# Wider token tiles for two FFNs behind a chunked attention, and a reordered start

## The reference

```python
# attention: q, k, v (4, 8, 768, 64); mem_k, mem_v (4, 8, 8, 64)
for c in range(S // 32):                       # chunks of 32 queries
    q_c = q[:, :, 32*c : 32*c + 32]
    k_ctx = k[:, :, max(0, 32*c - 16) : min(S, 32*c + 40)]     # v_ctx likewise
    k_full = concatenate([mem_k, k_ctx])                       # v_full likewise
    a = softmax(q_c @ k_full.T / 8)
    out[:, :, 32*c : 32*c + 32] = a @ v_full
x = out.transpose(0, 2, 1, 3).reshape(3072, 512)
# first FFN: 512 -> 2048 -> 512
r = maximum(x @ w_in, 0);  x = (s * r * r + b) @ w_out
# second FFN: 512 -> 2048 -> 512
h = x @ w_in2;             out = (h * sigmoid(1.702 * h)) @ w_out2
```

## Time and profile before

| | before |
|---|---|
| time, median of 3 runs | 1234.57 us (1234.47 to 1242.08) |
| time of the profiled execution | 1234.34 us |
| its span, first to last instruction | 1232.5 us |
| TensorE busy | 1221.0 us (99%) |
| VectorE busy | 611.5 us (50%) |
| ScalarE busy | 586.8 us (48%) |
| GpSimd busy | 231.4 us (19%) |
| HBM read, written | 46.14 MB, 12.58 MB |

### The profile page before, as it was taken

How to read it: one execution, slowest core, us unless ns; L and a number is a source line. 1 busy time by engine, 2 the same in 40 slices (tenths; PEclk the granted TensorE clock), 3 DMA queues, 4 the chain that set the end, 5 groups by cost and what they waited for, 6 DMA issues and landing times.

```text
span 1232.5 us, 20900 instructions
## 1 busy us (share of the span) xinstructions
PE 1221.0 (99%) x7124; PEld 1133.1 (92%) x7124; DVE 611.5 (50%) x2040; ACT 586.8 (48%) x1853; POOL 231.4 (19%) x248
## 2 busy tenths in 40 slices
PE   8999999999999999999999999999999999999998
PEld 5899999999999999988888999999999999999997
DVE  6776767766666777766444323323332332233222
ACT  6776666666565666656344422222232222232222
POOL 3864222332222222222045300000000000000000
PEclk9999999999999999999999999999999999999999
DMA  6751212121121132210143300001010000000000
GB/s 144 175 138 46 59 40 67 42 59 37 27 61 37 46 62 47 62 38 1 47 126 107 101 16 33 19 7 39 14 39 13 33 20 33 13 33 13 26 1 26
DMA packets 126094, 60.06 MB, mean 49 GB/s; under 512 B 94247, under 2 KB 118823, under 8 KB 125991
## 3 DMA queue, kind: packets, MB, share of 16 engines
q1 hardware_dynamic: 124768, 58.51, 18.9%
q10 hardware_dynamic: 1223, 0.23, 0.1%
HBM read 46.14 MB, written 12.58 MB: 48 GB/s over the span
## 4 chain that ended last, share of the span: by engine, by line
PE 98%; DVE 1%; ACT 1%; issue 0%; DMA 0%; POOL 0%; SPq 0%; DVEq 0%
PE psum L646 43%; PE psum L668 22%; PE psum L666 22%; PE psum L588 3%; PE psum L612 3%; PE psum L599 2%; PE psum L576 1%; PE psum L575 1%; PE psum L537 0%; PE psum L510 0%; PE psum L547 0%; DMA attn<-in_mem_k_dram 0%; PE psum L524 0%; DVE qk_lo L972 0%; PE psum L525 0%
## 5 line engine op out<-in xcount | busy, mean ns | idle before, releaser
L646 PE MATMUL psum<-x_hi,win_hi 128*128 128x384 f32 (+2 forms) x1024 | 352.1, 344 | 0.0
L646 PE MATMUL psum<-x_lo,win_hi 128*128 128x384 f32 (+2 forms) x1024 | 346.5, 338 | 0.0
L646 PE MATMUL psum<-x_hi,win_lo 128*128 128x384 f32 (+2 forms) x1024 | 345.2, 337 | 0.0
L646 PEld LDWEIGHTS psum<-x_hi,win_hi 128*128 128x128 f32 x1024 | 192.7, 188 | 8.4
L646 PEld LDWEIGHTS psum<-x_lo,win_hi 128*128 128x128 f32 x1024 | 192.5, 188 | 8.3
L646 PEld LDWEIGHTS psum<-x_hi,win_lo 128*128 128x128 f32 x1024 | 192.3, 188 | 3.6
L668 PE MATMUL psum<-g_hi,wout_lo 128*128 128x384 f32 (+2 forms) x512 | 173.8, 339 | 0.0
L668 PE MATMUL psum<-g_lo,wout_hi 128*128 128x384 f32 (+2 forms) x512 | 173.6, 339 | 0.0
L668 PE MATMUL psum<-g_hi,wout_hi 128*128 128x384 f32 (+2 forms) x512 | 172.7, 337 | 0.0
L817 ACT ACTIVATE g_hi<-ffn 128x384 fp32r<-128x384 f32 x128 | 67.2, 525 | 197.5 <-PE psum L666 196.3
L666 PE MATMUL psum<-wout_hi,g_hi 128*128 128x512 f32 x384 | 151.3, 394 | 0.0
(11 more groups left out here) (105 smaller groups left out, 1824.9 us busy)
## 6 DMA issues: line engine op xcount, KB each, us to landing
attn<-in_k_dram SPq DMA_DIRECT2D x31, 240.0 KB
attn<-in_v_dram SPq DMA_DIRECT2D x30, 240.0 KB
attn<-x_scratch SPq DMA_DIRECT2D x32, 192.0 KB, 2.4
attn<-in_q_dram SPq DMA_DIRECT2D x31, 192.0 KB
out_dram<-result SPq DMA_DIRECT2D x7, 768.0 KB, 3.5
result<-in_moe_w_in_dram SPq DMA_DIRECT2D x16, 256.0 KB, 3.0
result<-in_moe_w_out_dram SPq DMA_DIRECT2D x16, 256.0 KB, 2.8
attn<-in_moe_w_in_dram SPq DMA_DIRECT2D x16, 256.0 KB, 3.1
```

Of the source, the lines that this page charges most:

```text
L646: last = nc.tensor.matmul(dst, w[:, f, kt, :], x[:, mm % 2, kt, 0:n], start=(kt + i == 0), stop=(kt == KT - 1 and i == 2))
```

## The change

The first FFN has seven tiles (384, 384, 384, 480, 480, 480, 480), the second six of 512. The x buffers are 480 wide (`XMAX`), and in the second FFN `x_of` places four pieces of 512 in them from either end; every other tile's last piece lies where v was. A tile of 512 has four pieces in the second product, so all four accumulators are used and copied. With the new sizes the beats of tile 0 are 17, not 13, and they begin at place 56, not 48. In kind 1 `exp` and `invert` stand ahead of the two splits. Up front ScalarE splits q and k of unit 18 ahead of normalizing unit 16, GpSimd splits w_in of step 2 ahead of v, and the identity products are two of 512 columns and one of 128 in place of one of 512 ahead of the first transposes, and 384 columns in place of 256 in two rounds. Several small buffers are now parts of one. At the end ScalarE copies accumulator 3 whole, in place of half of accumulator 2.

```diff
--- before.py
+++ after.py
@@ -26,8 +26,8 @@
 MASKED = -3.0e38
 
 
-TILES = ((384, 288, 288, 384, 384, 384, 480, 480), (384,) * 8)
-TMAX = max(max(t) for t in TILES)
+TILES = ((384, 384, 384, 480, 480, 480, 480), (512,) * 6)
+XMAX, TMAX = max(TILES[0]), max(max(t) for t in TILES)
 M0 = len(TILES[0])
 MT = M0 + len(TILES[1])
 HALVES = TILES[0][0] // QT * 2
@@ -69,7 +69,7 @@
     for mm in range(M0):
         beats = beats_of(mm)
 
-        first, places = (48, 24 * (NF - 2)) if mm == 0 else (24 * NF * mm, 24 * NF)
+        first, places = (56, 24 * NF - 56) if mm == 0 else (24 * NF * mm, 24 * NF)
         for i, n in enumerate(beats):
             at.setdefault(first + places * i // len(beats), []).append((1, n))
             at.setdefault(first + places * (2 * i + 1) // (2 * len(beats)), []).append((2, n))
@@ -124,8 +124,8 @@
         win_lo = sb("win_lo", [P, NF, KT, P], F32R)
         wout_hi = sb("wout_hi", [P, NF, DM], F32R)
         wout_lo = sb("wout_lo", [P, NF, DM], F32R)
-        x_hi = sb("x_hi", [P, 2, KT, TMAX], F32R)
-        x_lo = sb("x_lo", [P, 2, KT, TMAX], F32R)
+        x_hi = sb("x_hi", [P, 2, KT, XMAX], F32R)
+        x_lo = sb("x_lo", [P, 2, KT, XMAX], F32R)
         ffn = sb("ffn", [P, 2, TMAX])
         g_hi = sb("g_hi", [P, 2, TMAX], F32R)
         g_lo = sb("g_lo", [P, 2, TMAX], F32R)
@@ -137,18 +137,12 @@
         pT_lo = sb("pT_lo", [P, 2, 2 * QT], F32R)
         v_hi = sb("v_hi", [P, 2, DM], F32R)
         v_lo = sb("v_lo", [P, 2, DM], F32R)
-        exp_bias = sb("exp_bias", [QT, 2, 2])
-        total = sb("total", [QT, 2, 2])
-        total_e = sb("total_e", [QT, 2])
-        inv_total = sb("inv_total", [QT, 2, 2])
-        s_bias = sb("s_bias", [QT, 2, 4])
-        s_total = sb("s_total", [QT, 2, 4])
-        s_total_e = sb("s_total_e", [QT, 4])
-        s_inv = sb("s_inv", [QT, 2, 4])
+        small = sb("small", [QT, 4, 2, 2])
+        exp_bias, total, inv_total, total_e = small[:, 0], small[:, 1], small[:, 2], small[:, 3, 0]
         ident = sb("ident", [P, P])
         masks = sb("masks", [QT, 3, P], BF16)
-        s_col = sb("s_col", [P, 1])
-        b_col = sb("b_col", [P, 1])
+        columns = sb("columns", [P, 2])
+        s_col, b_col = columns[:, 0:1], columns[:, 1:2]
 
         nonlin, gated = ffn[:, 0, :], ffn[:, 1, :]
 
...
@@ -262,6 +258,18 @@
             if part_of(mm):
                 return result[:, c * DM:(c + 1) * DM]
             return result[:, c * size_of(mm):(c + 1) * size_of(mm)]
+
+        def x_of(x, v, mm, kt):
+
+            n = size_of(mm)
+            if not part_of(mm):
+                return x[:, mm % 2, kt, 0:n]
+            every = x.rearrange("p a k t -> p (a k t)")
+            upper = (mm - M0) % 2 == (M0 - 1) % 2
+            if (mm - M0) % 2 == 0 and kt == KT - 1:
+                return v[:, 0, 0:n]
+            first = 2 * KT * XMAX - (KT - 1 if (mm - M0) % 2 == 0 else KT) * DM if upper else 0
+            return every[:, first + kt * DM:first + kt * DM + n]
 
         def mask_of(j):
             return 0 if j % QPB == 0 else 2 if j % QPB == QPB - 1 else 1
@@ -416,7 +424,7 @@
                         load_w_in(1, f)
                         load_w_out(1, f)
             for c in range(pieces_of(MT - 1)):
-                sp.wait_ge(result_copied[c], MT + (c == pieces_of(MT - 1) - 1))
+                sp.wait_ge(result_copied[c], MT)
                 sp.dma_start(out[start_of(MT - 1) + c * P:start_of(MT - 1) + (c + 1) * P, :],
                              result[:, c * DM:(c + 1) * DM]).then_inc(result_stored, 16)
             sp.wait_ge(result_stored, 16 * (MT - 1 + pieces_of(MT - 1)))
@@ -481,8 +489,8 @@
             split_w_in(0, 1)
             first_normalize(7)
             split_w_out(0, 1)
+            split_w_in(0, 2)
             split_v(FIRST // HP)
-            split_w_in(0, 2)
             for mm in range(MT):
                 for f in range(NF):
                     if mm == 0 and f + EARLY < NF:
@@ -541,7 +549,7 @@
             def first_transpose_probs(i):
                 if i:
                     pe.wait_ge(s_pT_ready, i)
-                keep_busy(s_bank_p, 1, 2)
+                keep_busy(s_bank_p, 1, 3 if i < 2 else 2)
                 pe.wait_ge(s_probs_ready, i + 1)
                 for h in range(4):
                     last = nc.tensor.transpose(s_bank_p[:, h * QT:(h + 1) * QT], s_probs[i % 2][:, h, :], ident[0:QT, 0:QT])
@@ -633,7 +641,8 @@
                 pe.wait_ge(w_in_ready, NF * part_of(mm) + f + 1)
                 dst = hid[f % 2][:, 0:n]
                 for kt in kts:
-                    for i, (w, x) in enumerate(((win_hi, x_hi), (win_hi, x_lo), (win_lo, x_hi))):
+                    xh, xl = x_of(x_hi, v_hi, mm, kt), x_of(x_lo, v_lo, mm, kt)
+                    for i, (w, x) in enumerate(((win_hi, xh), (win_hi, xl), (win_lo, xh))):
                         for g in AT.get(24 * step + 3 * kt + i, ()):
                             group(*g)
                         if f == 0 and i == 0:
@@ -643,7 +652,7 @@
                                 pe.wait_ge(s_x_ready, HALVES - 1 + kt // 2)
                             else:
                                 pe.wait_ge(x_ready, nth((first_unit(mm + 1) if mm + 1 < M0 else UNITS) - HP + kt))
-                        last = nc.tensor.matmul(dst, w[:, f, kt, :], x[:, mm % 2, kt, 0:n],
+                        last = nc.tensor.matmul(dst, w[:, f, kt, :], x,
                                                 start=(kt + i == 0), stop=(kt == KT - 1 and i == 2))
                 if kts[-1] == KT - 1:
                     last.then_inc(hid_ready, 1)
@@ -670,7 +679,8 @@
                         last.then_inc(last_rows_done, 1)
                 last.then_inc(g_used, 1)
 
-            keep_busy(s_bank_p, 1, 4)
+            keep_busy(s_bank_p, 2, 4)
+            keep_busy(s_bank_p, 1, 1)
             first_transpose(0)
             first_transpose(1)
             for r in range(HALVES):
@@ -786,12 +796,12 @@
 
             def group(kind, n):
                 if kind == 1:
+                    if there(n + 2):
+                        exp(n + 2)
                     if there(n + LEAD):
                         split_qk_hi(n + LEAD)
                     if there(n + 1):
                         split_pT_hi(n + 1)
-                    if there(n + 2):
-                        exp(n + 2)
                 else:
                     if there(n):
                         copy_x_hi(n)
...
@@ -871,8 +881,8 @@
             split_qk_hi(FIRST + 1)
             exp(FIRST)
             nonlinear(0, 0)
+            split_qk_hi(FIRST + 2)
             normalize(FIRST)
-            split_qk_hi(FIRST + 2)
             act.wait_ge(sb_loaded, 32)
             split_g_hi(0, 0)
             nonlinear(0, 1)
@@ -904,8 +914,7 @@
             act.wait_ge(result_stored, 16 * (MT - 1))
             nc.scalar.activation(result[:, 0:DM], acc[0][:, :], ACT.Copy).then_inc(result_copied[0], 1)
             act.wait_ge(g_used, NF * MT)
-            nc.scalar.activation(result[:, 2 * DM:2 * DM + DM // 2], acc[2][:, 0:DM // 2], ACT.Copy
-                                 ).then_inc(result_copied[2], 1)
+            nc.scalar.activation(result[:, 3 * DM:4 * DM], acc[3][:, :], ACT.Copy).then_inc(result_copied[3], 1)
 
         @block.vector
         def _(dve):
...
@@ -1008,12 +1017,12 @@
 
             def group(kind, n):
                 if kind == 1:
+                    if there(n + 2):
+                        invert(n + 2)
                     if there(n + LEAD):
                         split_qk_lo(n + LEAD)
                     if there(n + 1):
                         split_pT_lo(n + 1)
-                    if there(n + 2):
-                        invert(n + 2)
                 else:
                     if there(n + LEAD - 1):
                         mask_and_max(n + LEAD - 1)
...
@@ -1092,8 +1101,7 @@
                     for place in range(24):
                         if place == 0 and f == LAG and mm:
                             copy_result(mm - 1, 1)
-                            if part_of(mm - 1) == 0:
-                                copy_result(mm - 1, 3)
+                            copy_result(mm - 1, 3)
                         for kind in (1, 2):
                             for g in AT.get(24 * step + place - AFTER[kind], ()):
                                 if g[0] == kind:
@@ -1109,8 +1117,8 @@
             dve.wait_ge(last_rows_done, 2)
             dve.wait_ge(result_stored, 16 * (MT - 1))
             nc.vector.tensor_copy(result[:, DM:2 * DM], acc[1][:, :]).then_inc(result_copied[1], 1)
-            dve.wait_ge(result_copied[2], MT)
-            nc.vector.tensor_copy(result[:, 2 * DM + DM // 2:3 * DM], acc[2][:, DM // 2:DM]).then_inc(result_copied[2], 1)
+            dve.wait_ge(last_rows_done, 3)
+            nc.vector.tensor_copy(result[:, 2 * DM:3 * DM], acc[2][:, :]).then_inc(result_copied[2], 1)
 
 
 # ---- launch: one core; inputs and outputs as the reference has them ----
```

(6 more changed lines are left out.)

8 lines of the change are left out of this document (5 added, 3 removed).

## The result

The changed kernel takes 1219.2 us, median of 4 runs (1218.93 to 1219.22), where the kernel before takes 1234.58 beside it (1234.47 to 1242.08). The ratio is 0.9854, 95% interval 0.9814 to 0.9893: faster by 1.5%, 15.4 us. The profiled execution has a span of 1216.9 us and a time of 1218.93.

What follows compares the result with a forecast made beforehand. From about 42 us on, TensorE's matmul count times spacing, plus its waits, bounds the kernel. Span 1232.5 - 4.1 - 4.0 - 1.7 - 1.3 + 1.5 + 0 - 0.2 = 1222.7, time 1224.5 us, range 1220.5 to 1230.5.

Steps and rivals of the forecast that it cites:

- the term -4.1: Second FFN, 8 x 384 to 6 x 512: 532.2 us against 536.3, so -4.1 us, ends -6.4 and +1.2.
- the line through 384 and 480: Second FFN price: 0.429 ns a column plus 10.6 ns fixed a matmul, carried on to 512 gives 230.3 ns.
- the direct rows: Second FFN price: profile rows of nine 512-column matmuls taking 2.10 and 2.07 us, 231.7 ns each.
- the first (width buys nothing): Both FFNs: a matmul costs by the column, so 8.1 us stay out, giving 1232.6 us; chance 0.04.
- the fourth (a small fixed part): Both FFNs: fixed part of 1.8 ns, 768 fewer matmuls give 1.4 of the 8.1 us, hence 1231.2; chance 0.07.
- The start of step 2: First FFN's step 2 starts at about 40.5 us instead of 42.25: -1.7 us, ends -1.8 and 0.
- The wait of 1.15 us near 80 us: TensorE's wait for the normalization behind VectorE's addition was to go with the new order: -1.3 us, ends -1.3 and 0.
- the price of seven tiles: First FFN, eight tiles to seven, 384 fewer matmuls: -4.0 us, ends -4.2 and -1.9.
- +1.5 of waits: New waits in tile 0 with 17 units for 13, ScalarE at 92%: +1.5 us, ends 0 and +6.5.
- rival 2: Tile 0 becomes ScalarE's, every beat waiting for the normalization: 19.6 us in place of 1.5, 1242.6 us; chance 0.08.
- Up front: Longer identity products before the first transposes, faster clock winning back the loss: 0 us, ends +0.7 and -3.4.
- rival 3: The clock is up early and the whole start moves with it, -3.4 us: 1221.1 us; chance 0.20.

Runs made afterwards that it cites:

- the uniform streams: Kernel of nothing but matmul streams of one width, other engines idle, computing nothing of the reference: 173.3 ns a matmul at 384 columns, 216.7 at 480, 226.7 at 512.
- the old start: Changed kernel with before's order up front (normalization ahead of split, v ahead of step 2's w_in, first group at place 48): 1218.84 us, ratio 0.982.

## Why the prediction was wrong

**The step that failed is the price of a 512-column matmul, 231.0 ns.** It measured 226.7, and the term -4.1 became -14.1. Two sources agreed on about 231: the line through 384 and 480 (230.3) and the direct rows (231.7). The direct rows are from a stream that changes its width every nine or twelve matmuls, and its members carry the 0.07 us a step that this costs. The line fails on its own, and not only for its 384s from the same mixture: even the uniform streams, 173.3 at 384 and 216.7 at 480, give 231.1 when carried on, since 480 is dearer by the column (0.451 ns) than 512 (0.443). What could have been seen is that the only 512s of the trace stood in a mixture that the change ends; the forecast never asked what the mixing costs. Its range took -6.4 for the lower end of this term, from the quicker of two steps, which is a bound on the scatter and not on the mistake. Of the rivals, the first (width buys nothing) and the fourth (a small fixed part) looked for the error on the wrong side; the fixed part is 13.3 ns, more than the 10.6 of the forecast.

The Trainium skill, TensorE: Matmul & The Clock Gate, section Back-to-back issue gap, has 2.5 ns of fixed part for a single matmul by itself at full clock; for a stream it has about 131 ns at 512, which no run here shows. The uniform streams here have a fixed part of 13.3 at 384 and at 512, so the trace agrees with neither for this kind of matmul. Its 215.8 lay on the right side of the 231.7 of the mixed rows, but by another reason than the one found.

**The other terms.** The start of step 2 was right at its place (-1.8 against -1.7, with the gating late next) and worth nothing, as the old start showed. The wait of 1.15 us near 80 us is down to 0.23, at a row of the changed kernel's timeline from about the same time (with 17 beats for 13 it is another unit's):

```profile
79.60 0.39 PE L607 MATMUL psum<-ident,attn 96*128 96x96 f32 x2 [0.23 <-ACT attn L782]
```

VectorE's addition ahead of it still ran against a GpSimd subtraction, but earlier in the beat. The tile windows of the first FFN were forecast as 84.05, 88.1, 102.6, 103.6, 102.0 and 83.2 and came as 83.84, 87.83, 103.00 (293.84 to 396.84), 104.05, 101.93 and 83.30: within 0.5 us, and 0.4 in their sum. So the price of seven tiles was right, and tile 0 took it back. Tile 0 was to take 77.7 us with +1.5 of waits in it, and took 83.07, above the 82 that the forecast had named as a sign of being wrong: the mild form of rival 2. ScalarE's busy time came as worked out (69.8 us, measured 69.90). The reason was named, the normalization behind ScalarE's other work at a high load, but its price is 1.5 + 5.4 = 6.9 us, just above the upper end of +6.5; I had put it near the lower end because the new order removes one known cause, and that order turned out to be worth 0.9 us in this tile. Up front gave -1.3 where 0 was taken, by rival 3's means (the full rate by 7.5 us) at well under rival 3's size. The tail was a copy of 0.60 us, as taken.

The profiled span is 5.8 us under the forecast's 1222.7: -10.0 from the second FFN, +5.4 from tile 0, -1.3 up front, +0.4 from the other tiles and -0.3 from smaller ones. That it is no further off is luck: the two large errors have opposite signs.

## What to carry to other kernels

A price per instruction read from a mixed stream holds for that mixture alone: when a change makes the stream uniform, look for a uniform stretch at the same width, or widen the range by what the mixing may cost. When an engine at 84% load delays an urgent instruction, move the instruction that can wait to the other engine, not the urgent one. Time gained ahead of a stretch that another engine sets is not gained.
